# TensorE's experts 1 to 6 as a hardware loop, expert 0's rare tiles moved ahead of it, and the FFN's first block moved into the attention's last wait

## The chip, the core and the metric

The kernel runs on one core of a Trainium2 chip. A core has five engines with instruction streams of their own: TensorE (matmuls, PE in the profile, its weight loads PEld), VectorE (DVE), ScalarE (ACT), GpSimd (POOL) and SyncE (SP, which here only starts DMAs). They meet through semaphores. The metric is the device time of the program in microseconds, from which the median of several executions is taken.

## The reference, cut to what matters

```python
def _attn_ref(r, k, v, w, u):                    # B, H, S, D = 2, 8, 768, 48
    for t in range(S):
        kt, vt, rt = k[:, :, t], v[:, :, t], r[:, :, t]
        cur = einsum('bhd,bhe->bhde', u[None] * kt, vt)
        y[:, :, t] = einsum('bhd,bhde->bhe', rt, state + cur)
        state = w[None, :, :, None] * state + einsum('bhd,bhe->bhde', kt, vt)
...
def _moe_ref(x, w_in, w_out, alpha):             # 1536 tokens, 384 -> 2048 -> 384
    h = x @ w_in
    return (maximum(h, 0.0) + alpha * minimum(h, 0.0)) @ w_out
...
def _moe2_ref(x, w_gate, w1, w2, capacity):      # 8 experts, 384 -> 1024 -> 384
    logits = x @ w_gate; expert_idx = argmax(logits, axis=1)
    # softmax gives the token's gate; the first 384 tokens of each expert are kept
    h = maximum(einsum('ecd,edf->ecf', disp, w1), 0.0)
    y = einsum('ecf,efd->ecd', h, w2)
    # out[i] = gate_w[i] * y[expert_idx[i], pos[i]] for kept tokens, else 0
```

A linear attention with decay, then a dense feed-forward network (FFN, "mlp"), then a mixture of 8 experts ("moe") that takes each token to one expert.

## The kernel before

Every engine's program is written by hand, in one order, with hand-written semaphore waits; nothing schedules it. Three stages follow each other.

**Attention** goes over 12 tiles of 128 tokens (`for t in range(T)` on TensorE). Per tile it turns k (`k_turn`), makes the scores (`scored`), takes the state's part and then the scores' part of the output (`stage2`, lines 1318 and 1326) and updates the state (`update`). The scores' part waits until VectorE has masked the scores (`mask`, line 956), and VectorE until ScalarE has written their diagonals (line 676). The last tile's output is split into a high and a low part by `x_high` and `x_low`.

**FFN.** Every f32 product is made as three fp32r products of high and low parts: high with high, high with low, low with high. Tokens come in 4 groups of 384, the width of 2048 in 16 blocks of 128 (a block is a "chunk" of weights, with 384 columns of w_in and 384 of w_out). `up(g, f)` makes 9 matmuls (line 1359); VectorE makes the leaky relu in two operations (`leaky`, lines 1014 and 1020), ScalarE rounds it to the high part (`g_high`, line 705), GpSimd subtracts (`g_low`, line 551), and `down(g, f)` makes 9 matmuls (line 1374). In group 0 the weights are split too: ScalarE rounds a chunk (`split_high`, line 659), VectorE subtracts its two halves in two operations of `split_low` (line 933). GpSimd has split the first half of chunks 0 to 3 during the attention (EARLY = 4). Groups 1 to 3 are a loop on TensorE (`pe.Fori`), with a body of 316 matmuls.

**Experts.** While the last FFN group ends, 256 early rows of expert 0 go through `early_up` and `early_down`; expert 0 keeps up to 128 more rows. The number of rows of each expert stands in `counts`, and each engine reads it into a register (`rows_of`) and branches on it. An expert has three tiles of 128 rows, and there are three ways through it:

- at most 128 rows: `flip_up` twice (18 matmuls, 512 columns), `flip_turn` (8 transposes), the next expert's rows turned (`turn_xe`, 9 transposes), then `expert_down(e, 0)` with 24 matmuls (line 1593);
- up to 256 rows: `expert_ups` (8 blocks of 9 matmuls, 256 columns, line 1555, with the next expert's 9 transposes between), `expert_down(e, 1)` and `expert_down(e, 0)`;
- more: these and the third tile by `flip_up`, `flip_turn` and `expert_down(e, 2)`.

In this data expert 0 (after its early rows), 5, 6 and 7 go the first way, experts 1, 2 and 3 the second and expert 4 the third. On TensorE the code of all 8 experts is written out one after the other, each with both sides of two branches (If on 128 rows, If on 256 rows), 238 matmuls in an expert. After an expert's tiles, ScalarE scales its outputs by the gate (`y_copy`, line 828) and GpSimd scatters them to `out` with indirect DMAs (`y_scatter`, line 609). GpSimd waits for the scatters of the experts before (`s_out`) and then counts `s_gone` up, which frees `y_out` and `token`. The weights of expert e+2 are loaded and split while e and e+1 run; the first half by ScalarE and GpSimd (lines 798 and 633), the second by ScalarE and VectorE (lines 807 and 1145). The last three chunks of expert 1 (`split_high` and `split_low` of 29 to 31) are split at the end of expert 0's branch.

## Time and profile before

| | us |
|---|---|
| median of 3 runs | 434.99 |
| lowest, highest | 433.43, 435.9 |
| profiled execution, its own time | 433.0 |
| its span, first to last instruction | 431.3 |

The profile is of one execution. In its page, a digit row gives the busy share in 40 slices of the span; groups of instructions have the form "line engine op out<-in xcount | busy, mean of one | idle before, and who ended it".
### The profile page before, as it was taken

How to read it: one execution, taken by the hardware profiler on the slowest of the kernel's cores; microseconds unless marked ns; L12 is line 12 of the kernel's file. 1: busy time of each engine (PE TensorE's matmuls, PEld its weight loads, DVE VectorE, ACT ScalarE, POOL GpSimd, SP SyncE). 2: the span in 40 equal slices, each digit the busy share in tenths (PEclk: the TensorE clock that was granted, in tenths of full speed). 3: DMA queues.
4: the chain of work that ended last, by engine and by line, in shares of the span. 5: the costliest groups of instructions: out<-in, count | busy, mean ns of one | idle time of the engine just before them, and what ended most of it. 6: DMA issues, size and time to landing. Idle time of an engine off the chain costs nothing.

```text
span 431.3 us, 9203 instructions
## 1 busy us (share of the span) xinstructions
PE 407.6 (95%) x3200; PEld 389.3 (90%) x3200; DVE 263.5 (61%) x525; ACT 195.5 (45%) x446; POOL 228.2 (53%) x239
## 2 busy tenths in 40 slices
PE   5799999999999999999999999999699999999892
PEld 5698889999999999999999999987699999998672
DVE  6898867676436334353444796756586695726850
ACT  2889943433311114011142433425668777437840
POOL 3999725554322533126254593142939476437942
PEclk9999999999999999999999999999899999999997
DMA  6996035444990100001000455059575685817400
GB/s 244 403 370 217 3 82 165 131 135 152 362 358 3 53 2 0 0 0 55 0 0 4 129 154 171 18 144 388 176 254 161 234 258 185 277 25 244 140 29 10
DMA packets 34339, 61.89 MB, mean 144 GB/s; under 512 B 4798, under 2 KB 27310, under 8 KB 34288
## 3 DMA queue, kind: packets, MB, share of 16 engines
q1 hardware_dynamic: 31280, 55.92, 39.3%
q0 software_dynamic: 3008, 5.29, 3.6%
q8 instruction: 31, 0.51, 0.5%
q14 instruction: 20, 0.16, 0.1%
HBM read 47.92 MB, written 15.18 MB: 146 GB/s over the span
## 4 chain that ended last, share of the span: by engine, by line
PE 59%; PEld 15%; issue 7%; POOL 5%; DVE 5%; ACT 4%; DMA 2%; PEldq 0%; POOLq 0%; ACTq 0%; DVEq 0%
PE bank L1374 23%; PE bank L1359 23%; PEld bank L1593 7%; PEld bank L1555 6%; ACT scores L676 3%; POOL w_low L633 3%; PE bank L1480 2%; PE bank L1490 2%; DMA out<-y_out,token 2%; PEld bank L1617 1%; PE bank L1326 1%; DVE scores L956 1%; POOL out L609 1%; DVE w_low L1145 1%; PE bank L1617 1%
## 5 line engine op out<-in xcount | busy, mean ns | idle before, releaser
L551 POOL TENSOR_TENSOR g_low<-act_full,g_high 128x384 fp32r<-128x384 f32 x63 | 63.7, 1011 | 113.7 <-ACT g_high L705 113.7
L705 ACT ACTIVATE g_high<-act_full 128x384 fp32r<-128x384 f32 x64 | 33.7, 526 | 148.9 <-DVE act_full L1020 136.3
L1359 PE MATMUL bank<-x_split,w_high 128*128 (+1 forms) x384 | 98.3, 337 | 0.0
L1014 DVE TENSOR_SCALAR neg<-bank,alpha_sb 128x384 f32<-128x384 f32 x64 | 39.3, 614 | 78.0 <-PE bank L1359 78.0
L1359 PEld LDWEIGHTS bank<-x_split,w_high 128*128 128x128 f32 x384 | 69.0, 188 | 0.2 <-issue 0.2
L633 POOL TENSOR_TENSOR w_low<-w_raw,w_high 128x384 fp32r<-128x384 f32 x48 | 50.5, 1086 | 33.5 <-ACT w_high L798 33.5
L1374 PE MATMUL bank<-w_high,g_high 128*128 128x384 f32 x189 | 65.0, 344 | 0.0
L1359 PE MATMUL bank<-x_split,w_low 128*128 (+1 forms) x192 | 64.4, 336 | 0.0
L1374 PE MATMUL bank<-w_high,g_low 128*128 128x384 f32 x189 | 63.8, 338 | 0.0
L1374 PE MATMUL bank<-w_low,g_high 128*128 128x384 f32 x189 | 63.8, 337 | 0.0
L933 DVE TENSOR_TENSOR w_low<-w_raw,w_high 128x384 fp32r<-128x384 f32 x44 | 35.5, 812 | 10.5 <-ACT w_high L659 10.5
L1593 PE MATMUL bank<-w_high,expert_g_high 128*128 128x384 f32 x104 | 35.6, 342 | 2.9 <-DVE expert_g_low L1196 1.8
L1374 PEld LDWEIGHTS bank<-w_high,g_high 128*128 128x128 f32 x189 | 35.4, 187 | 2.1 <-POOL g_low L551 1.0
L1020 DVE SCALAR_TENSOR_TENSOR act_full<-bank,neg 128x384 f32<-128x384 f32 x64 | 35.7, 558 | 2.4
L1359 PEld LDWEIGHTS bank<-x_split,w_low 128*128 128x128 f32 x192 | 36.0, 188 | 0.0
L1374 PEld LDWEIGHTS bank<-w_low,g_high 128*128 128x128 f32 x189 | 35.5, 188 | 0.0
L1374 PEld LDWEIGHTS bank<-w_high,g_low 128*128 128x128 f32 x189 | 35.4, 187 | 0.0
L1593 PE MATMUL bank<-w_high,expert_g_low 128*128 128x384 f32 x104 | 34.8, 335 | 0.0
L1593 PE MATMUL bank<-w_low,expert_g_high 128*128 128x384 f32 x104 | 34.8, 335 | 0.0
L1145 DVE TENSOR_TENSOR w_low<-w_raw,w_high 128x384 fp32r<-128x384 f32 x48 | 33.0, 704 | 0.0
L609 POOL DMA_INDIRECT out<-y_out,token x24 | 26.0, 1082 | 12.5 <-DMA out<-y_out,token 6.7
L1555 PE MATMUL bank<-xe_high,w_high 128*128 128x256 f32 x96 | 28.5, 297 | 2.8 <-issue 2.8
(164 smaller groups left out, 846.3 us busy)
## 6 DMA issues: line engine op xcount, KB each, us to landing
w_raw<-chunks SPq DMA_DIRECT2D x96, 192.0 KB, 4.1
w_raw<-chunks SPq DMA_DIRECT2D x32, 384.0 KB, 3.5
rk_in<-att_rk SPq DMA_DIRECT2D x12, 704.0 KB, 6.4
routed_rows<-fill SPq DMA_DIRECT2D x1, 5211.0 KB, 16.8
xe<-routed_rows SPq DMA_DIRECT2D x7, 579.0 KB, 4.5
v_in<-att_v SPq DMA_DIRECT2D x12, 200.0 KB, 6.1
out<-fill SPq DMA_DIRECT2D x1, 2304.0 KB, 23.4
x_split<-x_split POOLq DMA_DIRECT2D x18, 48.0 KB, 2.5
```

Source lines behind the costliest of these rows:

```text
L551: pool.tensor_tensor(gl[:, f % 4, :], act_full[:, f % 2, :], gh[:, f % 4, :].bitcast(f32), ALU.subtract).then_inc(s_gl, 1)
L609: pool.indirect_dma_start(out=out, out_offset=bass.IndirectOffsetOnAxis(ap=token[:, e % 2, i:i + 1], axis=0), in_=y_out[:, e % 2, i, :], i ...
L633: pool.tensor_tensor(wl[:, slot, 0:W1], raw1[:, f, :], wh[:, slot, 0:W1].bitcast(f32), ALU.subtract).then_inc(s_wl1e, 1)
L705: act.activation(gh[:, f % 4, :], act_full[:, f % 2, :], ACT.Copy).then_inc(s_gh, 1)
L933: dve.tensor_tensor(wl[:, slot, part], raw[:, m, part], wh[:, slot, part].bitcast(f32), ALU.subtract).then_inc(s_wl1 if first else s_wl2, 1)
L1014: dve.tensor_scalar(neg[:, f % 2, :], h, 0.0, alpha_sb[:, f:f + 1], ALU.min, ALU.mult)\
L1020: dve.scalar_tensor_tensor(act_full[:, f % 2, :], h, 0.0, neg[:, f % 2, :], ALU.max, ALU.add)\
L1145: dve.tensor_tensor(wl[:, slot, W1:CW], raw2[:, f, :], wh[:, slot, W1:CW].bitcast(f32), ALU.subtract).then_inc(s_wl2, 1)
L1359: last = mm(bank[f % 4][:, 0:G], a[:, f, w], x[:, kc, bass.ds(g * G, G)], start=kc == 0 and i == 0, stop=kc == KC - 1 and i == 2)
L1374: last = mm(bank[4 + i][:, 0:DM], a[:, f % 4, i * P:(i + 1) * P], w[:, slot, W1:CW], start=f == 0 and m == 0, stop=f == n - 1 and m == 2)
L1555: last = mm(bank[f % 4][:, 0:n], a[:, slot, w], x[:, e % 2, kc, 0:n], start=kc == 0 and i == 0, stop=kc == KC - 1 and i == 2)
L1593: last = mm(bank[4 + i][:, 0:DM], a[:, f, i * P:(i + 1) * P], w[:, s % SLOTS, W1:CW], start=f == 0 and m == 0, stop=f == NFE - 1 and m == 2)
```

## The change

1. **FFN's first block.** On TensorE `up(0, 0)` moves from behind the attention to before `stage2` of its last tile. On VectorE, the first-half split of chunk f+4, done after block f, becomes that of chunk f+3, from block 1 on.
2. **Expert 0.** Its second and third tile, which it has only with more than 128 rows left, get code of their own in front (`flip_up`, `flip_turn` and a new `flip_down` for each), behind one branch that this data skips. Its first tile then stands outside any branch. The rows of tiles 1 and 2 are turned only in the rare branch. The splits of chunks 29 to 31 move ahead of `flip_high` on ScalarE and between the two `flip_relu` on VectorE, and `keep_meta(0)` (the copies of tokens and gates) ahead of the branch.
3. **Loop.** Experts 1 to 6 on TensorE become three turns of a loop over two experts; expert 7 stands behind it. Row numbers are read at the head of each expert (`rows_of`), no longer in `early_down`. Waits now compare with register values.
4. **`flip_down`** takes the place of `expert_down` for a flipped tile and for tile 0 of experts with up to 256 rows: in each half first the 8 products with the high part of g, then the 4 with its low part.
5. **Last scatter.** GpSimd no longer waits for the scatters of experts 0 to 6 before those of expert 7.

```diff
             def load_xe(e):
                 if e >= 2:
-                    sp.wait_ge(s_te, (e - 1) * GT)
+                    sp.wait_ge(s_te, (e - 2) * GT + 1 if e > 2 else 2)
...
-                if e:
+                if 0 < e < E - 1:
                     pool.wait_ge(s_out, e * 16 * GT)
                     pool.sem_inc(s_gone, 1)
...
+            for c in range(2 * NF - 3, 2 * NF):
+                split_high(c)
+            flip_high(0, 0, (0,))
+            xe_high(1, 0, bank[X_BANK[0]])
+            flip_high(0, 0, (1,))
...
-                    if split == "mlp" and f + EARLY < NF:
-                        split_low(f + EARLY, first=True)
+                    if split == "mlp" and EARLY < f + EARLY <= NF:
+                        split_low(f + EARLY - 1, first=True)
...
+                if t == T - 1:
+                    pe.wait_ge(s_par, 32)
+                    pe.wait_ge(s_cast, 1)
+                    pe.wait_ge(s_moved, MOVES)
+                    pe.wait_ge(s_masked, T - 1)
+                    up(0, 0)
                 stage2(t)
...
+            def flip_down_high(e, i, half, b):
+                pe.wait_ge(s_fc[i], 2 * e + half + 1)
+                for f in range(half * HF, (half + 1) * HF):
+                    pe.wait_ge(s_wl2, s + NF + 1)
+                    for w in (wh, wl):
+                        mm(bank[4 + i][:, 0:DM], egh[:, f, i * P:(i + 1) * P], w[:, b * NFE + f, W1:CW],
+                           start=f == 0 and w is wh, stop=False)
...
             early_down(1, 0)
             pe.wait_ge(s_cnti, 2)
-            rows = []
+            rows_0 = rows_of(pe, 0)
             for f in range(1, NFE):
-                rows.append(rows_of(pe, f - 1))
                 early_down(1, f)
-            rows.append(rows_of(pe, E - 1))
...
+            def expert(e, b):
+                rows = rows_of(pe, e)
+                with pe.If(rows < P + 1):
...
+            pe.wait_ge(s_wl1, NF + 2 * NFE)
+            with pe.Fori(1, E - 1, 2) as e:
+                expert(e, 1)
+                expert(e + 1, 0)
+            expert(E - 1, (E - 1) % 2)
```

How instructions stand now. TensorE at the attention's last tile, before: the state's part and the scores' part of tiles 10 and 11, then the FFN's first block.

```order
L1318 MATMUL bank<-r_hat,state 64x128 x8
L1326 MATMUL bank<-scores,v_in 64x128 x8
L1318 MATMUL bank<-r_hat,state 64x128 x8
L1326 MATMUL bank<-scores,v_in 64x128 x8
L1359 MATMUL bank<-x_split,w_high 128x384 x2
```

And now, at the same place:

```order
L1354 MATMUL bank<-r_hat,state 64x128 x8
L1362 MATMUL bank<-scores,v_in 64x128 x8
L1378 MATMUL bank<-x_split,w_high 128x384 x2
L1378 MATMUL bank<-x_split,w_low 128x384
...
L1354 MATMUL bank<-r_hat,state 64x128 x8
L1362 MATMUL bank<-scores,v_in 64x128 x8
```

The nine matmuls of `up(0, 0)` now stand between tile 10's output and both parts of tile 11's.

VectorE in expert 0, the branch that this data takes, before (L933 is `split_low` of chunks 29 to 31):

```order
L1190 TENSOR_SCALAR expert_g_by_token<-bank 128x512
L1151 TENSOR_TENSOR xe_low<-bank,xe_high 128x3x128
L1159 CAST token<-xe 128x3
L1160 COPY gate<-xe 128x3
L1190 TENSOR_SCALAR expert_g_by_token<-bank 128x512
L1196 TENSOR_TENSOR expert_g_low<-bank,expert_g_high 128x4x128
L1151 TENSOR_TENSOR xe_low<-bank,xe_high 128x3x128
L1196 TENSOR_TENSOR expert_g_low<-bank,expert_g_high 128x4x128
L1151 TENSOR_TENSOR xe_low<-bank,xe_high 128x3x128 x2
L933 TENSOR_TENSOR w_low<-w_raw,w_high 128x384 x3
```

And now (L953 is `split_low`):

```order
L1214 TENSOR_SCALAR expert_g_by_token<-bank 128x512
L953 TENSOR_TENSOR w_low<-w_raw,w_high 128x384 x3
L1214 TENSOR_SCALAR expert_g_by_token<-bank 128x512
L1220 TENSOR_TENSOR expert_g_low<-bank,expert_g_high 128x4x128
L1174 TENSOR_TENSOR xe_low<-bank,xe_high 128x3x128
L1220 TENSOR_TENSOR expert_g_low<-bank,expert_g_high 128x4x128
L1174 TENSOR_TENSOR xe_low<-bank,xe_high 128x3x128 x2
L1182 CAST token<-xe 128x3
```

The three splits went from behind both halves of g into the middle between them, and the copies of expert 0's tokens out of this stretch.

TensorE at the loop's end and the start of expert 7 behind it:

```order
L1792 UNCONDITIONAL_BRANCH
L1802 REGISTER_ALU
L1802 COMPARE_AND_BRANCH
L321 TENSOR_LOAD counts
L321 ISA x2
L1768 COMPARE_AND_BRANCH
L1701 MATMUL bank<-w_high,xe_high 128x512
```

The load of a row number now stands right in front of the branch that uses it, at the head of each expert; TensorE's program has four such loads, where before it had eight in `early_down`.

## Rows read from the trace of the kernel before

**Rows 1.** The page, section 1: busy us, share of the span, instructions

```profile
PE 407.6 (95%) x3200; PEld 389.3 (90%) x3200; DVE 263.5 (61%) x525; ACT 195.5 (45%) x446; POOL 228.2 (53%) x239
```

**Rows 2.** Windows from:to, us; busy PE, PEld, DVE, ACT, POOL; PEclk; DMA; GB/s

```profile
306.90:310.70 3.80, 3.76 (x19) 3.79 (x20) 1.34 (x2) 0.80 (x2) 3.80 (x5) 0.57 0.66 196
...
326.30:344.10 17.80, 17.80 (x130) 17.80 (x129) 13.40 (x25) 13.33 (x33) 11.44 (x12) 1.00 0.70 221
```

**Rows 3.** Timeline of PE at the attention's end: start, us, line, operation, idle before

```profile
55.92 1.09 PE L1318 MATMUL bank<-r_hat,state 64*64 64x128 f32 x16
58.07 1.09 PE L1326 MATMUL bank<-scores,v_in 128*64 128x128 f32 x16 [1.05 <-DVE scores L956]
59.09 0.62 PE L1359 MATMUL bank<-x_split,w_high 128*128 128x384 f32 x2
```

**Rows 4.** The chain that ended last, in FFN group 0: start, us, what

```profile
59.16 8.01 PE bank L1359 x45
67.17 5.02 PE bank L1374 x27
...
73.75 1.62 PE bank L1374 x9
...
105.63 1.59 PE bank L1374 x9
```

**Rows 5.** Timeline of DVE, then of ACT, in FFN blocks 0 and 1

```profile
61.03 0.62 DVE L1014 TENSOR_SCALAR neg<-bank,alpha_sb 128x384 f32<-128x384 f32 x1 [0.51 <-PE bank L1359]
...
63.69 0.62 DVE L933 TENSOR_TENSOR w_low<-w_raw,w_high 128x384 fp32r<-128x384 f32 x1 [0.98 <-ACT w_high L659]
...
62.81 0.85 ACT L659 ACTIVATE w_high<-w_raw 128x768 fp32r<-128x768 f32 x1
```

**Rows 6.** Timeline of PE in `early_down`, around two reads of row numbers

```profile
284.25 0.33 PE L1490 MATMUL bank<-w_high,expert_g_low 128*128 128x384 f32 x1
284.58 0.41 PE L1490 MATMUL bank<-w_high,expert_g_high 128*128 128x384 f32 x1
```

**Rows 7.** Timeline of PE at the start of expert 0

```profile
289.37 0.82 PE L1522 MATMUL bank<-ident,xe 128*128 128x128 f32 x6
...
291.59 0.47 PE L1617 MATMUL bank<-w_high,xe_high 128*128 128x512 f32 x1 [0.35 <-DVE xe_low L1151]
```

**Rows 8.** Timeline of PEld from expert 0's down products to expert 1

```profile
298.32 0.19 PEld L1593 LDWEIGHTS bank<-w_high,expert_g_high 128*128 128x128 f32 x1 [0.40 <-issue]
...
302.82 0.19 PEld L1593 LDWEIGHTS bank<-w_high,expert_g_high 128*128 128x128 f32 x1 [1.40 <-issue]
...
306.91 0.19 PEld L1555 LDWEIGHTS bank<-xe_high,w_high 128*128 128x128 f32 x1 [3.10 <-issue]
```

**Rows 9.** DMA queues, window 160 to 266 us (all three), then 300 to 303 us

```profile
q1 hardware_dynamic: 1598, 4.03, 13.5%
q0 software_dynamic: 384, 1.19, 2.9%
q14 instruction: 1, 0.01, 0.0%
...
q8 instruction: 1, 0.02, 2.2%
```

**Rows 10.** Timeline of PE, first matmul of expert 6

```profile
401.50 0.47 PE L1617 MATMUL bank<-w_high,xe_high 128*128 128x512 f32 x1 [1.25 <-issue]
```

**Rows 11.** Timeline of PE, first down products of experts 6 and 7

```profile
408.56 0.41 PE L1593 MATMUL bank<-w_high,expert_g_high 128*128 128x384 f32 x1 [0.68 <-DVE expert_g_low L1196]
...
419.18 0.41 PE L1593 MATMUL bank<-w_high,expert_g_high 128*128 128x384 f32 x1 [0.66 <-DVE expert_g_low L1196]
```

**Rows 12.** Timeline of ACT and of POOL at the end

```profile
423.72 0.58 ACT L828 ACTIVATE y_out<-bank,gate 128x384 f32<-128x384 f32 x1 [3.54 <-PE bank L1593]
...
425.43 0.97 POOL L609 DMA_INDIRECT out<-y_out,token  x1 [0.31 <-issue]
```

**Rows 13.** Timeline of DVE, the splits of chunks 29 to 31

```profile
300.51 3.93 DVE L933 TENSOR_TENSOR w_low<-w_raw,w_high 128x384 fp32r<-128x384 f32 x3
```

361 lines of the change are left out of this document (219 added, 142 removed).

## The prediction

> **What bounds the kernel now.** I read the shares of the engines first, then windows over the stages, the chain that ended last, and the timelines at each place that the diff touches. TensorE is busy 95% of the span, the next engine 61% [rows 1]. In a stage without gaps it is busy all the time: expert 2 keeps it for 17.80 of 17.80 us, with VectorE at 13.40, ScalarE at 13.33, GpSimd at 11.44 [rows 2]. So the time is TensorE's work plus TensorE's gaps, and behind it the last scatter. The change removes hardly any matmul; what it can win is the gaps. The gaps of about half a microsecond or more on the path are: the wait for the last mask [rows 3], two reads and a handover around expert 0 [rows 6, 7], three gaps with no releaser but "issue" [rows 8, 10], and waits of the flipped experts for the low part [rows 11]. Each other engine has slack, so a shift of TensorE's work carries on to the end unless one of the rivals below holds it.
>
> **The FFN's first block.** TensorE ends the state's part of tile 11 at 57.0 and waits until 58.07 for the mask [rows 3]. `up(0, 0)` costs 45 matmuls / 8.01 us, so 1.6 us for 9 [rows 4]. Put in front at 55.9, it ends at 57.5, the state's part (1.0) at 58.5: the scores' part starts 0.4 later than the 58.07 of before. One block of 1.6 less, 0.4 later: 1.2 won by there, if the block's inputs are in; its weights and its tokens have been ready for microseconds. Then VectorE: `leaky(0)` stood at 61.03, behind the split of the last tile's output, and can't be much earlier. Block 4's first-half split ended at 64.3 (63.69 + 0.62) [rows 5]; now it stands behind `leaky(1)` and another split, at about 65.0, and `up(4)`, ready to start at 64.3, waits for it. It starts 0.6 earlier than before (65.0 against 67.17 - 1.56). So 0.6 by block 4. After that the cycle of before goes: VectorE waited 0.98 for ScalarE's rounding of the same chunk [rows 5] in every block, and TensorE's down products came at 1.62 us per 9 there against 1.59 at the group's end [rows 4]. 10 blocks at 0.03, and the 27 products of 5.02 that need only 27 x 0.177 = 4.8: 0.5 more. **1.2 us** in all (1.1 to 1.3 by either way of counting; 0 if the wait that takes the place of the old one is as long as the block).
>
> **Reads of row numbers.** TensorE's matmuls of 384 columns follow at 0.17 us, but 284.25 to 284.58, across a read, is 0.33 [rows 6]. The first reads hide behind queued work, the last four show 0.16 to 0.2 each, and one at the end 0.3: **0.8 us** gone. They come back at the head of six loop experts and of expert 7. One read and its branch against a queue of work that, by the way the first four hide, is about a microsecond deep: I take 0.1 each, **0.5 us** in all; the ends are 0 and 0.6 each (0.77 us per block with a read, less 6 instructions that take a part of it), 4.2 in all. The Trainium skill ("Runtime: NRT & Kernel Launch", section "Instruction fetch mechanics") puts a register load at some 200 ns; by that figure, as an estimate, seven unhidden reads would be 1.4 us. The sum stays with the rows.
>
> **Expert 0's start.** Six transposes stood before the last six early products, 0.82 us [rows 7]; three stay: 0.3. Expert 0 began at 291.59, 0.5 after the last product, because it waited for both tiles' low parts [rows 7]; for one tile the wait is about 0.2: 0.3. Three more transposes go in its middle (0.4). Against that, VectorE makes the three splits between the halves of g. They took 3.93 us for three beside GpSimd [rows 13], 0.55 each alone. The second half's relu then comes 0.6 to 2 us after TensorE has run out of transposes. I take 0.6, net of the 0.4: 0.2 lost. Together **0.4 us** won; at the long splits 1 lost.
>
> **Code gaps.** PEld stood still 1.40 us in the middle of expert 0's down products and 3.10 before expert 1 [rows 8]. The last split that expert 1 could wait for ended at 304.4 [rows 13], and the gap at 301.4 to 302.8 had no input outstanding. In the first a packet of the instruction queue q8 lies just before the restart [rows 9]. I read these as blocks of code that had not come. After them the granted clock was 0.57 for 3.80 us [rows 2], a loss of 0.43 x 3.8 = 1.6. The same kind of gap, 1.25, stands before expert 6 [rows 10]. What tells whether the change removes them: a block is 16 KB; a matmul is two instructions [rows 1], and expert 0 jumped over 105 matmuls into a block, ran through its rest in 2 to 4 us while the weights of expert 2 were loading, and jumped on. By my count of the code the next block was asked for only at the first jump. In the changed kernel the jump comes 8 us earlier, before expert 0's tile, so the next block has 10 us to come; then each block of the loop is in use for 5 us or longer in the first turn. And in turns two and three nothing need be fetched: FFN groups 2 and 3 run from 160 to 266 us and q8 moves nothing at all in them, only a single packet of q14 [rows 9], though their body has 316 matmuls. The expert body has 476, half as much again. Gone: 1.1 + 2.9 + 1.6 = 5.6 and 1.25 before expert 6: **6.9 us**.
>
> The skill's same section says the opposite of what this change banks on: that instruction memory is a short sequential buffer with no benefit from locality, and that a taken branch out of its window stalls. The trace does not agree with it for 316 matmuls [rows 9]; for 476 no row here tells, and the rule is the rival for slower below. The same section gives TensorE's memory as 128 KiB, eight such blocks, which would hold the body.
>
> **High products first.** Before, the flipped experts' down products waited for VectorE's low part: 0.68 and 0.66 us [rows 11], and 0.27 in expert 5. Now eight products of high parts (1.4 us) come first, and ScalarE's part is ready 0.7 earlier. **1.6 us.** Nothing is late in its place: the low part is there 0.7 into the 1.4.
>
> **The end.** The last y tile is copied at 423.72 to 424.30, the last scatter begins 1.1 later [rows 12], since GpSimd was held by the wait for expert 6's scatters. Without that the scatter needs about 0.8 from the copy to its start: **0.3 us.** GpSimd's own row of scatters (1.28 each) could bind when TensorE ends some 3 us earlier relative to it; by my count it is 0 to 0.5 us from doing so.
>
> **Sum**, against the profiled execution's 433.0 us (span 431.3, 1.7 around it): -1.2 - 0.8 + 0.5 - 0.4 - 6.9 - 1.6 - 0.3 = -10.7, so 422.3. That execution lay 2 us under the median of the runs shown, 434.99; a gain of 2.5% puts the median at **424.2 us**.
>
> **Rivals.**
>
> *The code gaps stay, at other places.* Two jumps in a row are still there, with weights loading, at the entry of the loop and at the exit to expert 7. For it: before, three of the eleven such places stalled, all with weights loading. Against it: the count of code above. If the 6.9 stay whole: 424.2 + 6.9 = 431.1. If one gap of 2.9 stays with its clock loss: 428.7.
>
> *The loop's bookkeeping shows.* Seven reads at 0.6 and a register operation for each wait: 424.2 + 3.7 = 427.9. For it: every wait in the body now has such an instruction, often one for two matmuls. Against it: FFN groups 1 to 3 use such waits with no gap, if fewer of them.
>
> *The other engines don't follow.* VectorE's splits beside GpSimd at 1.3 us each cost expert 0 another 1.4 [rows 13] and the front block wins nothing (1.2): 424.2 + 2.6 = 426.8.
>
> *Slower: the body doesn't stay in instruction memory.* It is half as long again as the one that does. Then each return to the top is a jump to a block that isn't there, and the next jump, over the short branch, to another. From [rows 8], a landing costs 3.10; two are 6.2, and 1.6 for the clock: 7.8 per return, 15.6 for two, against 6.9 banked, and the forward jumps of later turns stall as well where they now don't. 424.2 + 15.6 = 439.8. It decides as soon as the engine keeps fewer than the five or six blocks of this body; four are shown. This is the mechanism that ends above the time of before.
>
> **How the numbers follow.** Forecast 0.58; gaps at other places 0.13; bookkeeping 0.11; others don't follow 0.08; slower 0.10. A measurement of this kernel tells about 0.5% (2.2 us) from no change. The forecast's own range, from the bounds of the reads, the splits and the block, is 421.5 to 427; the rivals short of the slower one reach 431.1. Leaving out the slower one and the full stay of the gaps gives 421.2 to 430.5. Faster by over 0.5%: the first four cases less a little for two of them meeting, 0.87; same 0.04; slower 0.09.
>
> **What would show it.** In the changed profile: the FFN's chain begins with 36 matmuls of the up line behind the last scores' part, and its down groups read 1.59 early on; the products of `early_down` follow at 0.17 without gaps but one; no "issue" gap over 0.5 us on PEld between expert 0 and expert 1 and no window there below clock 1.00; no packet of q8 between the loop's second turn and its end; the first product of flipped experts' downs waits under 0.2 us; the last scatter begins under 0.9 us after the last copy. The prediction is wrong if q8 is busy in turns two and three, or if "issue" gaps stand at each expert's head, or if a DVE line ends TensorE's waits in expert 0 for over a microsecond.

## The result, and the profile after

| | before | after |
|---|---|---|
| median of 14 runs, us | 435.14 (433.43 to 435.9) | 431.12 (429.56 to 433.11) |
| profiled execution, us | 433.0, span 431.3 | 429.56, span 427.9 |
| granted clock, mean | 0.991 | 0.996 |

The ratio is 0.9925, with a 95% interval of 0.9911 to 0.994. The change is 0.75% faster; 2.5% were forecast. The direction was right, the size was not: 431.12 lies outside the range of 421.2 to 430.5.

The page's first section after, as [rows 1] of before, and the row of instruction packets from the page's third (queue, kind: packets, MB, share):

```profile
PE 406.9 (95%) x3194; PEld 388.8 (91%) x3195; DVE 258.3 (60%) x523; ACT 192.6 (45%) x442; POOL 229.8 (54%) x239
...
q8 instruction: 22, 0.36, 0.3%
```

TensorE has six transposes fewer. Its busy time falls by 0.7 us and its idle time by 2.7 (431.3 - 407.6 = 23.7 us before, 427.9 - 406.9 = 21.0 after). Where the 3.4 us went is read from the first product of each expert in TensorE's timelines:

| first product of | before | after | ahead of before |
|---|---|---|---|
| expert 0 | 291.59 | 289.65 | 1.94 |
| expert 1 (two tiles) | 306.94 | 300.91 | 6.03 |
| expert 2 (two tiles) | 326.45 | 318.85 | 7.60 |
| expert 3 (two tiles) | 344.36 | 338.33 | 6.03 |
| expert 4 (three tiles) | 362.31 | 357.82 | 4.49 |
| expert 5 (one tile) | 389.43 | 386.51 | 2.92 |
| expert 6 (one tile) | 401.50 | 397.13 | 4.37 |
| expert 7 (one tile) | 412.79 | 409.85 | 2.94 |
| span's end | 431.3 | 427.9 | 3.4 |

Up to expert 2 the forecast is nearly kept: 7.6 us won. Then each of experts 2, 3 and 4 gives back some 1.55 us, and in expert 6 another 1.43 of the 1.45 that its start had won goes. The first product of experts 1 and 3, and of the down in expert 2 (TensorE's timeline: start, duration, line, operation, idle before):

```profile
300.91 0.28 PE L1600 MATMUL bank<-xe_high,w_high 128*128 128x256 f32 x1
...
329.88 0.44 PE L1631 MATMUL bank<-w_high,expert_g_high 128*128 128x384 f32 x1 [0.55 <-DVE xe_low L1174]
...
338.33 0.28 PE L1600 MATMUL bank<-xe_high,w_high 128*128 128x256 f32 x1
```

Ahead of expert 1 there is no gap any more, where before there were 3.10 [rows 8]. But from expert 1 to 2 are 17.94 us, from 2 to 3 19.48 and from 3 to 4 19.49, where before the last two were 17.91 and 17.95 (the first was 19.51, with the lower clock of [rows 2] in it). What stands before expert 2's relus is seen on ScalarE. First before, in the same place one expert later, then after (ScalarE's timeline; the first row of each is `flip_high` of the expert that ends, the last the first relu of the next):

```profile
339.87 1.09 ACT L843 ACTIVATE expert_g_high<-bank 128x512 fp32r<-128x512 f32 x2 [2.73 <-PEq L1681]
340.84 1.77 ACT L798 ACTIVATE w_high<-w_raw 128x384 fp32r<-128x384 f32 x4
...
345.63 0.38 ACT L790 ACTIVATE expert_g_high<-bank 128x256 fp32r<-128x256 f32 x1
```

```profile
315.91 1.09 ACT L848 ACTIVATE expert_g_high<-bank 128x512 fp32r<-128x512 f32 x2 [4.31 <-PEq L1791]
316.88 1.77 ACT L801 ACTIVATE w_high<-w_raw 128x384 fp32r<-128x384 f32 x4
...
321.58 0.40 ACT L793 ACTIVATE expert_g_high<-bank 128x256 fp32r<-128x256 f32 x1
```

Before, the relu starts 1.27 us behind the next expert's first product (345.63 - 344.36), which is about when its block is made. After, it starts 2.73 us behind it (321.58 - 318.85). What released `flip_high` is line 1791, `pe.sem_inc(s_ft[2], 2)`: a count which says that the third tile's halves are turned, raised without work where there is no third tile (line 1681 before, where the same count was `s_ft[1]`). Before, TensorE raised it after 15 of the 24 products of the first tile's down. The change rewrote the down as `flip_down` and put the count behind all 24:

```diff
-                    expert_down(e, 0, range(HF + 1))
-                    pe.wait_ge(s_mgl, e * NFE + NFE + C_MGL)
-                    pe.sem_inc(s_ft[1], 2)
-                    expert_down(e, 0, range(HF + 1, NFE))
+                    flip_down(e, 0, b)
+                    pe.sem_inc(s_ft[2], 2)
```

Nine products of 0.173 us are 1.56 us. In a two-tile expert ScalarE runs `flip_high(e, 2)` all the same, on data nobody uses, and behind it stand its splits of the next W1 and its copies of y: 5.67 us (315.91 to 321.58) from there to the next relu. The late count of one two-tile expert so delays the relus of the expert behind it: those of experts 1, 2 and 3 lengthen experts 2, 3 and 4.

### The profile page after: what moved, and what is told of

The parts are those of the page before. It is cut to its first block, busy times and chain, and to the rows that moved or that the text cites. A ratio compares the mean times of both kernels' runs of the same rounds, so it can differ in the third digit from the quotient of the medians.

```text
span 427.9 us, 9352 instructions
## 1 busy us (share of the span) xinstructions
PE 406.9 (95%) x3194; PEld 388.8 (91%) x3195; DVE 258.3 (60%) x523; ACT 192.6 (45%) x442; POOL 229.8 (54%) x239
## 4 chain that ended last, share of the span: by engine, by line
PE 69%; DVE 9%; issue 5%; PEld 5%; POOL 4%; DMA 3%; ACT 2%; SPq 0%; PEldq 0%; POOLq 0%; ACTq 0%; DVEq 0%
PE bank L1417 24%; PE bank L1378 23%; POOL w_low L636 4%; PE bank L1362 3%; PE bank L1701 3%; DVE w_low L1165 3%; PE bank L1326 3%; PE bank L1354 2%; PE bank L1651 2%; PE bank L1631 2%; PEld bank L1600 2%; PEld bank L1631 2%; DMA w_raw<-chunks 2%; PE bank L1312 1%; DVE expert_g_low L1158 1%
## 5 line engine op out<-in xcount | busy, mean ns | idle before, releaser
L554 POOL TENSOR_TENSOR g_low<-act_full,g_high 128x384 fp32r<-128x384 f32 x63 | 65.2, 1035 | 111.2 <-ACT g_high L708 111.2
L1165 DVE TENSOR_TENSOR w_low<-w_raw,w_high 128x384 fp32r<-128x384 f32 x48 | 33.5, 714 | 0.0
L953 DVE TENSOR_TENSOR w_low<-w_raw,w_high 128x384 fp32r<-128x384 f32 x44 | 31.2, 736 | 0.2 <-ACT w_high L662 0.2
L679 ACT ACTIVATE scores<-ident,diag 128x128 f32<-128x128 f32 x96 | 29.4, 398 | 2.4 <-DVE diag L968 2.4
L662 ACT ACTIVATE w_high<-w_raw 128x768 fp32r<-128x768 f32 x32 | 26.8, 838 | 2.6 <-DMA w_raw<-chunks 2.6
L1600 PE MATMUL bank<-xe_high,w_low 128*128 128x256 f32 x96 | 27.1, 282 | 0.0
```

Source lines behind the costliest of these rows:

```text
L554: pool.tensor_tensor(gl[:, f % 4, :], act_full[:, f % 2, :], gh[:, f % 4, :].bitcast(f32), ALU.subtract).then_inc(s_gl, 1)
L662: act.activation(wh[:, slot, :], raw[:, m, :], ACT.Copy).then_inc(s_wh, 1)
L679: last = act.activation(scores[:, t % 2, h % 2, h // 2, :], ident[:, :], ACT.Copy, scale=diag[:, t % 2, h:h + 1])
L953: dve.tensor_tensor(wl[:, slot, part], raw[:, m, part], wh[:, slot, part].bitcast(f32), ALU.subtract).then_inc(s_wl1 if first else s_wl2, 1)
L1165: dve.tensor_tensor(wl[:, slot, W1:CW], raw2[:, f, :], wh[:, slot, W1:CW].bitcast(f32), ALU.subtract).then_inc(s_wl2, 1)
L1600: last = mm(bank[f % 4][:, 0:n], a[:, slot, w], x[:, b, kc, 0:n], start=kc == 0 and i == 0, stop=kc == KC - 1 and i == 2)
```

## The experiments

Ratios are to the kernel before, run beside each group on the same chip. Spans and starts are of each kernel's profiled execution.

**x1: the count first.**

```diff
-                    no_tile(2)
-                    flip_down(e, 0, b)
-                    pe.sem_inc(s_ft[2], 2)
+                    pe.sem_inc(s_ft[2], 2)
+                    no_tile(2)
+                    flip_down(e, 0, b)
```

> Theory A (a count that comes too late): in the changed kernel TensorE raises the count for the third tile's halves (s_ft[2]) of a two-tile expert after all 24 products of the first tile's down, nine products of 0.17 us later than the kernel before did; ScalarE's copies, its split of the next W1, GpSimd's half of that split, VectorE's keep_meta and so the next expert's first relu stand behind it. Here the count is raised ahead of those 24 products. By A the distance between the starts of two-tile experts falls from 19.5 to about 17.9 us for experts 2, 3 and 4, and the whole run is 3 x 1.6 = 4.7 us shorter than the change: 426.4 us, range 424 to 428, a ratio of 0.980 to the kernel before. Rival B (the loop's registers: TensorE computes its waits from registers in every turn, and that costs the 1.6 us per expert): nothing moves, 431 us, and the starts stay 19.5 us apart. Rival C (the two-tile experts wait for the weights' load or split, not for this count): 431 us too, with the wait of VectorE's keep_meta gone but one of a weight's in its place.

Measured 427.06 us, ratio 0.9805 (0.9776 to 0.9833), span 424.4. The distances are 17.94, 17.91 and 17.95. By the two ratios the one line moved gives 1.2% of the time; by that of x5 below, which executes the same instructions and came to 0.9848, it gives 0.8%. Either is as much as the whole change had. ScalarE at the end of expert 2:

```profile
330.02 1.09 ACT L848 ACTIVATE expert_g_high<-bank 128x512 fp32r<-128x512 f32 x2 [0.57 <-PEq L1789]
```

It starts 6.66 us ahead of expert 3's first product (336.68), where after it started 2.94 ahead of expert 2's. Expert 3's first relu then starts 1.27 us behind the first product, as in the kernel before, and now ScalarE waits 0.40 for TensorE there: 1.27 is the earliest that it can be. Rivals B and C fall. Not all of the gain lasts: x1 is 4.76 us ahead of the changed kernel at expert 5 (381.75 against 386.51) and 3.5 at the span's end, because expert 6 takes 13.61 us in x1 and 12.72 in the changed kernel. x6 below says why.

**x2: the kernel before with the count last.**

```diff
-                    expert_down(e, 0, range(HF + 1))
-                    pe.wait_ge(s_mgl, e * NFE + NFE + C_MGL)
-                    pe.sem_inc(s_ft[1], 2)
-                    expert_down(e, 0, range(HF + 1, NFE))
+                    expert_down(e, 0)
+                    pe.sem_inc(s_ft[1], 2)
```

> The kernel before with nothing changed but the place of the same count: after all 24 products of the first tile's down instead of after 15. Theory A: experts 2, 3 and 4 take 1.6 us more each, so 435.1 + 4.7 = 439.8 us (438 to 441), ratio 1.011, with the starts of the two-tile experts about 19.4 us apart instead of 17.9. Rival B (the loop's registers) and rival C (weights): no change, 435.1 us.

Measured 439.56 us, ratio 1.0078 (1.0058 to 1.0098). The distances from 2 to 3 and 3 to 4 are 19.42 each. So the late count costs the old kernel as well, with no loop in it. The three experts take 1.51, 1.47 and 1.53 us more, 4.5 together; the medians differ by only 3.1. The kernel before was at 436.45 in this group of runs and at 434.4 to 435.3 in the others, so what the medians say is itself known to a microsecond or so only; no run says more of the rest.

**x3 and x4: no loop**, with the count last and first.

```diff
-            with pe.Fori(1, E - 1, 2) as e:
-                expert(e, 1)
-                expert(e + 1, 0)
-            expert(E - 1, (E - 1) % 2)
+            for e in range(1, E):
+                expert(e, e % 2)
```

> The change with its loop written out (each expert's code stands once, with constants in its waits), all else kept, the late count too. Theory A: the two-tile experts' starts stay 19.5 us apart, and the three stops for code and the clock drop come back: +6.9 us less what the waits behind the late count take of them (up to 3 us), so 435 to 438 us, ratio 1.000 to 1.007. Rival B: the registers' cost goes with the loop, the two-tile experts take 17.9 us again and the code gaps come back: 431.1 - 4.7 + 6.9 = 433.3 us.

> The loop written out and the count raised ahead of the 24 products. Theory A: against the first run of this set (426.4) only the code stops come back, +6.9 us: 433.3 us (431.5 to 434.5), ratio 0.996; the difference of this run and the first is the value of the loop by itself. If the loop's worth is less than forecast (the stops for code were in part cover for other waits), this one comes out at 430 or lower. Rival B: the same 433.3, but then the first run stays at 431, so that the loop is worth only 2 us.

Measured 432.4 us, ratio 0.9923 (0.9896 to 0.9949), and 426.9 us, ratio 0.9793 (0.9771 to 0.9816). Forecast were 435 to 438 us and 433.3. Both are as fast as their partners with the loop (0.9925 and 0.9805). This is the surprise of the study: the forecast's largest term was put down to the loop, and the loop is not needed for most of it. The trace of x4 has no stop before expert 1, whose first product is at 301.66, right behind expert 0's last, and the clock stays at 1.00. Of the three stops of before only the one ahead of expert 6 is there:

```profile
395.23 0.47 PE L1701 MATMUL bank<-w_high,xe_high 128*128 128x512 f32 x1 [1.77 <-POOL w_low L636]
```

This row names GpSimd's split, but x1's expert 6, with the same splits, starts without a wait; two instruction packets of x4 lie in these microseconds, none of x1. Nor was the split late. The eight splits of expert 6's first half end with this row of GpSimd's timeline in x4, at 386.03, 7 us before the stop begins (393.46):

```profile
384.01 2.02 POOL L636 TENSOR_TENSOR w_low<-w_raw,w_high 128x384 fp32r<-128x384 f32 x2 [0.34 <-ACT w_high L801]
```

I read it as a stop for code under a wrong name. The loop's own worth is 0.7 us of span (425.1 against 424.4), and nothing that the timing can tell. Its registers cost nothing: expert 1 takes 17.94 with them, 17.93 without. The reads at the experts' heads cost nothing either: experts 2 and 3 take 17.91 and 17.95 in x1, with a read in front of each, as in the kernel before, which has none there. A window from 340 to 410 us of the changed kernel holds these DMA queues and no q8, whereas x4's same window holds eight packets of it (and five of q14):

```profile
q1 hardware_dynamic: 7967, 11.02, 51.4%
q0 software_dynamic: 704, 1.05, 4.0%
q14 instruction: 4, 0.03, 0.2%
```

```profile
q8 instruction: 8, 0.13, 0.8%
```

So the loop's body is not fetched again. Only, the fetches had been nearly free.

**x5 and x9: code that is never run, laid into expert 0** of x1's kernel. x5 had the condition `rows_0 < 0`, which was decided when the program was built, so its blocks were left out: 427.31 us, ratio 0.9848 (0.9822 to 0.9874), and nothing learned of code. But it shows what one program does in two executions, since x5 and x1 run the same 9352 instructions: ratios of 0.9848 and 0.9805, spans of 425.4 and 424.4, a wait in expert 0 of 1.46 us and of 0.59, and 18.17 us from expert 2 to 3 and 17.91. A difference of a microsecond between two spans is therefore no finding here. x9:

```diff
             flip_turn(0, 0, (1,))
+            with pe.If(rows_0 < P + 1):
+                pe.wait_ge(s_tel, 1)
+            with pe.Else():
+                keep_warm(105)
             flip_down(0, 0)
+            with pe.If(rows_0 < P + 1):
+                pe.wait_ge(s_tel, 1)
+            with pe.Else():
+                keep_warm(74)
```

> The first run of the study (loop kept, count raised first) with two stretches of code that is never run laid into expert 0: 105 transposes between its second turn and its down, 74 transposes between its down and expert 1. The kernel before jumps over as much code at these two places. Theory D (where expert 0's rare code stands, not the loop, took the two stops and the clock's drop away, as the run without the loop suggests: it has no stop there): both stops come back, about 1.1 us before expert 0's down and 2.9 us before expert 1, and expert 1 runs 1.6 us longer at the lower clock, +5.6 us on 427.1: 432.7 us (430.5 to 433.5), ratio 0.993. Rival E (it is the loop that took them away, by the code that it brings in or keeps): no change, 427.1 us, ratio 0.981.

> The fifth run again, with a condition that is only known when the program runs (the fifth one's could be decided when it was built, so its two blocks were left out of the program): in expert 0 of the first run's kernel TensorE now jumps over 105 transposes ahead of its down and over 74 behind it. Theory D (the place of the code in front of these two points made the two stops of the kernel before): 1.1 us before the down and 2.9 us before expert 1 come back, with the clock's drop behind them 5.6 us: 432.7 us, ratio 0.993. Rival E (what made them was something else of expert 0's old form, or the loop took them away): 427 to 427.5 us, ratio 0.982.

x9 took 440.12 us, ratio 1.0117 (1.0077 to 1.0157): 13 us more than x1, where 5.6 were forecast, though all that it executes besides is two tests and two waits that hold at once. The first product of expert 1 and the first of expert 7's down, and the clock behind the first stop and at the second (windows; busy PE, PEld, DVE, ACT, POOL; PEclk, DMA, GB/s):

```profile
306.35 0.38 PE L1600 MATMUL bank<-xe_high,w_high 128*128 128x256 f32 x1 [3.30 <-POOL w_low L636]
...
423.89 0.66 PE L1651 MATMUL bank<-w_high,expert_g_high 128*128 128x384 f32 x1 [4.02 <-issue]
```

```profile
306.90:310.30 3.40, 3.40 (x18) 3.40 (x17) 0.97 (x2) 0.92 (x3) 2.95 (x4) 0.50 0.77 219
...
422.90:429.70 6.80, 5.81 (x18) 5.84 (x19) 0.00 (x0) 0.58 (x1) 1.12 (x2) 0.50 0.02 3
```

The stop before expert 1 and the half clock behind it are back (the one before expert 0's down is not). A stop of 1.31 has come before expert 2, and one of 4.02 in expert 7, whose code nobody touched but which now lies elsewhere, with 6.8 us at half clock from within it. Against x1, expert 0 takes 4.9 us more, expert 1 3.1 and expert 7 6.0. The loop is in both kernels, so it is not what decides; that it is the place of code and not the two tests themselves, the next pair shows.

**x13 and x14: the kernel before, with never-run code some 20 us ahead of expert 0.**

```diff
                 early_down(1, f)
+                if f == 2:
+                    with pe.If(rows[0] < P + 1):
+                        pe.wait_ge(s_cnti, 2)
+                    with pe.Else():
+                        keep_warm(102)
```

> The kernel before with nothing changed but never-run code (102 transposes and the branch around them, 208 instructions) laid between two of its early downs, some 20 us ahead of expert 0, so that all code behind it lies 208 instructions further on. Theory D2 (the stops depend on where the jumps fall among the packets of instructions, about 256 instructions each by the profile's count of packets and MB, not on the loop or the order): by the distances, expert 0's second jump then no longer leaves the packet it starts in, so the stop before expert 1 (2.81 us) and the clock's drop behind it (1.6 us) go: 435 - 4.4 = 430.5 us (429 to 432), ratio 0.990. Rival E2 (the old form of expert 0 makes the stops wherever it lies): both stops stay, 435 us, ratio 1.000.

> The same with 51 transposes (106 instructions). By theory D2 both jumps of expert 0 still leave the packet that they start in, as in the kernel before, so the stops stay: 435 us, ratio 0.997 to 1.004; stops of other experts may shift. If the stop goes here as well, the distance of the packets isn't what decides, and some other property of the shift is. Rival E2: 435 us.

With 102 transposes: 433.41 us, ratio 0.9953 (0.9934 to 0.9972). With 51: 441.07 us, ratio 1.012 (1.0101 to 1.014). In the first, forecast at 430.5, the 2.81 before expert 1 are 0.71 and the clock doesn't drop, as expected; the 1.11 in expert 0's down are gone too, which was not; but new stops stand before a down of expert 1 (0.88), in expert 2 (0.89) and before expert 3 (0.59), so only a part is won. In the second I expected no change and was wrong: stops of 2 us and more at four places, of which one, expert 0's down, had 1.11 before and the others (in experts 5, 6 and 7) had none for code. Three of the four:

```profile
301.81 0.41 PE L1593 MATMUL bank<-w_high,expert_g_high 128*128 128x384 f32 x1 [3.23 <-issue]
...
400.50 0.33 PE L1593 MATMUL bank<-w_high,expert_g_high 128*128 128x384 f32 x1 [2.91 <-issue]
412.13 0.41 PE L1593 MATMUL bank<-w_high,expert_g_high 128*128 128x384 f32 x1 [3.40 <-DVE w_low L1145]
```

Both execute the same, a branch and a wait more than the kernel before, and differ only in how many never-run transposes lie there: 433.4 against 441.1 us. That the place of code decides is shown. The rule by which I placed it (a stop where a jump leaves its packet soon after the last one did) got one of the two right, and that one in part, and stays a guess.

**x6, x7 and x8: VectorE's order.** `keep_meta(e)` stood at the end of expert e-1 and waits there for GpSimd's scatters. x6 (count first) and x7 (count last) move it into expert e; x8 is x6 with the splits between two relus put behind both.

```diff
                         for i in range(1, GT):
                             xe_low(e + 1, i, bank[X_BANK[i]])
+                    if e > 1:
+                        keep_meta(e)
...
-                if e < E - 1:
-                    keep_meta(e + 1)
```

x8 has besides:

```diff
                     flip_relu(e, 0, 0)
-                    low2(0, 1)
                     flip_relu(e, 0, 1)
-                    low2(2)
+                    low2(0, 1, 2)
```

> Count raised first, and VectorE's keep_meta(e) moved from the end of expert e-1 into expert e (behind its halves' low parts in a one-tile expert, behind the eight relus in a two-tile one), from expert 2 on. In the trace of the first run VectorE stands 1.09 us before keep_meta ahead of expert 6 and takes 0.81 and 1.06 us for it, and TensorE's wait for its relu (1.21 us) follows. Theory A extended (keep_meta is the gate by which the scatter holds the relus): 1.2 us of TensorE's wait in expert 6 go and some of the 0.85 us: 425.6 us (424.5 to 426.5), ratio 0.977. Rival F (VectorE's weight splits, not keep_meta, bound experts 5 to 7): no change, 427 us.

> The change as it was measured, the count raised after the 24 products as there, with keep_meta(e) moved into expert e. Theory A says that the late count costs time only by way of keep_meta: VectorE's next relu stood behind it. So with the count late and keep_meta out of the way the starts of the two-tile experts should come back from 19.5 to about 17.9 us, and the time to that of the run before this one, within 0.5 us: 425.6 to 426.5 us, ratio 0.978. Rival G (the late count holds something else also, ScalarE's copy or GpSimd's split of the weights, which TensorE needs itself): 428 to 431 us, with starts 18.5 to 19.5 us apart.

> As the sixth run (count first, keep_meta later), and in one-tile experts, expert 0 among them, VectorE's weight splits that stood between its two relus (three in expert 0, two in the others) follow both relus. TensorE waited for the second relu 0.59 us in expert 0 and 0.85 us in expert 6 in the first run's trace, where these splits took 2.12 us. If VectorE's order bounds these experts, 1 to 1.5 us more go: 424.4 us (423.5 to 425.5), ratio 0.974. If the splits are then late for the next product that reads them, the same as the sixth run.

x6: 426.93 us, ratio 0.9834 (0.9803 to 0.9866), span 423.5 against x1's 424.4. Expert 6 takes 12.02 us instead of 13.61, so the wait was real, but the timing can't tell the 0.9 us (425.6 us were forecast). x8: 425.47 us, ratio 0.9788 (0.9771 to 0.9805), span 423.2, where 424.4 us were forecast. x7 corrects my theory: 429.62 us, ratio 0.9894 (0.9864 to 0.9924), distances of 19.02 and 19.04. With the count last and `keep_meta` out of the way only 0.45 of the 1.55 us per expert come back. So ScalarE's own queue is the main way in which the late count acts: in x7's expert 2 VectorE's first `relu_low` (which makes the low part of g) waits 4.19 us for ScalarE's relu.

```profile
324.35 0.42 DVE L1158 SCALAR_TENSOR_TENSOR expert_g_low<-bank,expert_g_high 128x256 fp32r<-128x256 f32 x1 [4.19 <-ACT expert_g_high L793]
```

**x17 and x18: how much of the delay counts.** x17 is the change with the count after 20 of the 24 products (between `flip_down_high(e, 0, 1, b)` and `flip_down_low(e, 0, 1, b)`); x18 is the kernel before with it ahead of all 24.

> The change with the count raised after 20 of the 24 products (the last four, the second half's low parts, follow it) instead of after 24. If ScalarE's queue sets the distance product by product, each of the starts of experts 3, 4 and 5 comes 4 x 0.173 = 0.69 us sooner after the one before (18.8 us instead of 19.5), 2.1 us in all: 431.1 - 2.1 = 429.0 us, ratio 0.9876 (0.985 to 0.990). If a threshold decides (a DMA caught or missed), the distance is either 17.9 or 19.5 us.

> The kernel before with the count raised ahead of the 24 products instead of after 15 of them. In its trace ScalarE's first relu of expert 3 starts 1.27 us after the expert's first product, which is 0.2 us later than in the first run's kernel, and TensorE does not wait: the count came just in time. So nothing is gained: 435.3 us, ratio 0.997 to 1.003, starts 17.9 us apart as before. If it gains over 1 us, the count was holding the kernel before too.

x17: 430.0 us, ratio 0.9888 (0.9865 to 0.9911), distances 18.80 and 18.83: 0.68 us less for four products of 0.173. x18: 435.29 us, ratio 1.001 (0.9992 to 1.0028), distances 17.92 and 17.95: nothing. Both as expected. (The expectation calls the relu 0.2 us later than in x1; x1 has the same 1.27.) The cost over 17.91 us is 1.57 behind 24 products, 0.89 behind 20 and nothing behind 15 or ahead of all. At 0.173 each that puts the last place that costs nothing, by estimate, at the 15th, and from there on each product is paid in full, once per expert.

**x10, x11 and x15: a one-tile expert's down inside the branch of its turns.** In x10 the product rows follow the turns without a second test of the row count. A two-tile expert's first tile takes `expert_down` again in all three. x11 adds x8's moves; x15 is x11 with 70 never-run transposes as in x13.

```diff
                     flip_turn(e, 0, (1,))
+                    pe.sem_inc(s_w1free, 1)
+                    pe.sem_inc(s_fh[2], 2)
+                    pe.sem_inc(s_ft[2], 2)
                     no_tile(1)
+                    no_tile(2)
+                    flip_down(e, 0, b)
                 with pe.Else():
...
-                with pe.If(rows < 2 * P + 1):
+                    with pe.If(rows < 2 * P + 1):
```

> The first run's kernel with a one-tile expert's down written inside the same branch as its turns, instead of behind a second test of the row count (the two-tile and the three-tile ways stand in the other branch). In the first run's trace TensorE idles 0.71 to 0.74 us between the last turn and the first product of the down in experts 6 and 7, and 0.38 us in expert 5, though the halves' high parts are there; in expert 0, whose down follows without a branch, no such gap shows. Theory H (the gap is the branch and the register waits behind it): 0.38 + 0.74 + 0.71 = 1.8 us less, of which the low parts of the halves may take back up to 0.8: 425.6 us (425 to 426.5), ratio 0.977. Rival I (the gap is ScalarE's copy of the first half): 427 us.

> The tenth run's kernel with the eighth's two moves on VectorE as well (keep_meta in the expert itself, the splits behind both relus). If the waits that each takes away are separate ones, their gains add up: 427.1 - 1.8 - 2 = 423.3 us, ratio 0.970 (422.5 to 424.5). If experts 5 to 7 are bound by the same chain in both, 424.5 to 425.5 us as the eighth.

> The eleventh run's kernel with 70 never-run transposes at the same place, so that the jumps of experts 1 and 2 leave a packet once instead of twice. Theory D2: the stop of 1.27 us before expert 2 goes and nothing else changes: 426.55 - 1.3 = 425.2 us, and its span 422.9 instead of 424.2. If another stop appears, the same or more.

x10: 427.06 us, ratio 0.9828 (0.9796 to 0.986), where 425.6 were forecast. The gap before the down, 0.53 in expert 7 of the changed kernel and 0.71 in x1, is 0.20 now (0.39 in expert 6); but the new code has a stop of 2.32 before expert 2, in the loop's first turn only. The first product of expert 7's down in the changed kernel and in x10, and x10's expert 2:

```profile
416.10 0.41 PE L1651 MATMUL bank<-w_high,expert_g_high 128*128 128x384 f32 x1 [0.53 <-issue]
```

```profile
323.29 0.38 PE L1600 MATMUL bank<-xe_high,w_high 128*128 128x256 f32 x1 [2.32 <-POOL w_low L636]
...
415.41 0.41 PE L1651 MATMUL bank<-w_high,expert_g_high 128*128 128x384 f32 x1 [0.20 <-issue]
```

x11: 426.55 us, ratio 0.9819 (0.9784 to 0.9854), stop of 1.27 at the same place, span 424.2; the two forecasts, 423.3 and 424.5 to 425.5, both fail. x15: 425.08 us, ratio 0.9771 (0.9752 to 0.9791), span 422.9: the stop is gone, and the 1.3 us of span are what was expected, if hardly more than the 1.0 between x1 and x5. It is the fastest of the study, 2.3% under the kernel before and, by the ratios, 1.5% under the change. x8, without any of this, is within its interval.

**x12: x1 without the FFN's part.** The first up block stands behind the attention again and VectorE's splits a block earlier, as before.

> The first run's kernel without the FFN's part of the change (the first up block stands behind the attention again, and VectorE splits W1 a block earlier). In the trace after the change the FFN's second group starts 0.84 us earlier than before. If that lasts to the end, this one takes 0.8 us more than the first run: 427.9 us, ratio 0.9825 (0.980 to 0.985), with group 1's first product at 107.2 instead of 106.4. Rival: the FFN's downs wait for something else, and nothing is lost, 427.1 us.

Measured 426.95 us, ratio 0.9823 (0.9784 to 0.9861): with such an interval the timing says nothing of 0.8 us, nor does the span, 425.0 against 424.4. In the traces the FFN's group 1 starts at 107.62 against 106.55 (106.86 in x5) and expert 0 at 290.87 against 289.81 (290.13), so there the block's gain is seen.

**x16: x1 with the plain order of products** in the loop and expert 7 (`expert_down(e, 0, b)` for `flip_down(e, 0, b)`).

> The first run's kernel with the plain order of products (high, low, low in turn) in experts 5 to 7; expert 0 keeps the new order. The forecast gave the new order 1.6 us in all, of 0.66 to 0.68 us waits before a down and one at expert 0. The trace after the change shows 0.4 to 0.7 us before the same downs still. If the order is worth its forecast, this one takes 0.27 + 0.68 + 0.66 = 1.6 us more, 428.7 us; if the gap is the branch and not the data (theory H), nothing changes: 427.1 us, ratio 0.9805.

Measured 428.41 us, ratio 0.9853 (0.9825 to 0.9882), span 425.7 against 424.4. The number is near the 428.7 that a full worth of the order gives, but the trace doesn't bear that out. The gap at expert 6's down is what it was with the new order:

```profile
403.27 0.44 PE L1631 MATMUL bank<-w_high,expert_g_high 128*128 128x384 f32 x1 [0.74 <-DVE expert_g_low L1220]
```

Of the 1.3 us 0.76 arise in expert 0, whose code is the same in both kernels, and the rest in experts 2 to 4, not at the places where I had put it. x5, with the new order, has just these longer times in experts 0 and 2 to 4, and its span is only 0.3 us under x16's. So the order is worth 0.5 us at most, and perhaps nothing.

## Why the prediction missed

The sum again, term by term, with what the traces show (us, minus is a gain).

| term | forecast | measured | |
|---|---|---|---|
| FFN's first block | -1.2 | -0.8 | group 1 starts at 106.38, not 107.22 |
| reads, and expert 0's start | -0.8, part of -0.4 | -1.1 | 1.94 at expert 0's start less the 0.8 |
| reads at the experts' heads | +0.5 | 0 | 17.91 and 17.95 in x1 as before |
| stops at expert 0 and the clock | -5.6 | -5.7 | 4.09 in expert 0, 1.57 in expert 1 |
| stop before expert 6 | -1.25 | -1.45, then +1.43 | VectorE's waits take its place |
| high products first | -1.6 | 0 to -0.5 | |
| the end | -0.3 | -0.3 to -0.5 | 1.38 from last copy to last scatter, not 1.71 |
| the count raised later | no term | +4.7 | 1.57, 1.54 and 1.57 in experts 2, 3 and 4 |

**The step that failed is one that is missing.** The list of edits called the new down an order of products. The same lines also moved a count from behind 15 products to behind 24, and neither the description nor the prediction has it. "Nothing is late in its place" was said of the low part, on TensorE alone. Who waits for TensorE was not asked. The trace of before had what was needed: ScalarE's `flip_high` released by that line after 2.73 us, 5.76 us from there to its next relu with no idle time between, and that relu 1.27 us after the expert's first product. There was no room. "Each other engine has slack" was read from ScalarE's share, 13.33 of 17.80 us [rows 2], and not at this place. With the term in it the sum is -6.0 instead of -10.7, and 424.2 + 4.7 = 428.9. Of the 2.2 us that are still missing, expert 6 has 1.2, the order of products 1.1 or more and the FFN's block 0.4, less the 0.5 for reads that cost nothing. One of the rivals, that the gaps for code stay at other places in full, gives 431.1 us, which is what was measured. That is chance: in this kernel those gaps are gone, and the count took their gain.

**High products first** was mis-sized. The 0.68 and 0.66 of [rows 11] name VectorE's low part, and I took the name for the cause. In x16 and x1 the gap at expert 6 is 0.74 with either order; in x10, where the second test of the row count no longer lies in it, it is 0.20 at expert 7 and 0.39 at expert 6. I read it so that the low part arrived while the branch was still being worked off: two things ended there at nearly the same time, and the row names one.

**The stop before expert 6** went as forecast, and nothing came of it. VectorE had been just behind: `keep_meta(6)`, held by the scatters, then the relu, then two splits between the relus. After, TensorE waits for the relus of expert 6:

```profile
401.88 0.63 PE L1722 MATMUL bank<-ident,expert_g_by_token 128*128 128x128 f32 x4 [0.46 <-DVE expert_g_by_token L1214]
...
404.28 0.66 PE L1722 MATMUL bank<-ident,expert_g_by_token 128*128 128x128 f32 x4 [0.79 <-DVE expert_g_by_token L1214]
...
405.56 0.44 PE L1651 MATMUL bank<-w_high,expert_g_high 128*128 128x384 f32 x1 [0.62 <-DVE w_low L1165]
```

x6 and x8 take that chain away, and expert 6 takes 12.02 and 12.06 us in them, not the 13.61 of x1. x4 shows it the other way round: with the 1.77 stop back ahead of expert 6, experts 5 and 6 together take 24.34 us, and 24.43 in x1 without it. The prediction asked what is late next for the products, not for this stop.

**The FFN's block** won 0.84 of 1.2. `up(4)` waits for VectorE as said and starts at 65.07, 0.54 earlier than before; 0.6 was forecast. Behind it 0.30 came of 0.5. The rows are of the chain that ended last, as [rows 4]:

```profile
56.19 1.77 PE bank L1378 x9
...
65.07 1.86 PE bank L1378 x9
66.93 4.77 PE bank L1417 x27
...
73.26 1.59 PE bank L1417 x9
```

The 27 products take the 4.77 that were worked out (5.02 before), and the blocks' downs 1.59 each (1.62 before). What the sum forgot is that `up(4)`, having to wait, takes 1.86 us for the 1.56 of its neighbours.

**What held.** The three stops were read as code that had not come; x9, which brings the one before expert 1 back by code that is never run, bears that out. The 5.6 us around expert 0 came to 5.7. The reason given for the two at expert 0 (the jump comes 8 us earlier, so that the next block has time) did not need the loop, and x3 and x4 agree with it; but x13 and x14 say that it is one lucky place among others. The rival that the code gaps go to other places, given 0.13, is no rival of this kernel but the general case: x9, x10, x11 and x14 each met it. The loop's bookkeeping cost nothing. The slower rival fell: 476 matmuls of loop body are fetched once and then kept, no packet of q8 from the second turn on. The rule of the Trainium skill ("Runtime: NRT & Kernel Launch", section "Instruction fetch mechanics"), that the memory is a short sequential buffer with nothing to gain from locality, doesn't hold for this loop on TensorE; the 128 KiB that the same section gives for TensorE's memory leave room for the body, and the trace agrees. Its warning that a taken branch out of the window stalls the engine fits the stops of x9 and x14, 1.3 to 4.0 us each; but x4 jumps over the unused branches of every expert and stops once.

**Expert 0's splits.** The wait for the second relu was put at 0.6. It is 0.83 in the changed kernel and between 0.59 and 1.73 in kernels with the same code there (x1, x4, x9, x10, x16); x1 and x5, the same instructions twice, have 0.59 and 1.46. x8, which has the splits behind both relus, has 0.33 before the first product of the down and no wait between the halves. Such a spread is itself larger than several terms of the sum, and no run says where it comes from.

## What to carry to other kernels

When an edit rewrites a stretch of an engine's program, list every semaphore that the stretch raises and the product after which it did so before and does now; then read from the other engine's timeline how much work it has between that count and the next thing the first engine needs. A wait that is removed pays only if the engine which would be late next has slack at that very place. A gain or a loss of one or two per cent from an edit that also moves code should be checked against the same kernel with never-run code laid ahead, before it is put down to the edit.

## What the runs showed of the hardware

- Code that is never run, by its amount, changed the time of one kernel from 435.3 to 433.4 or 441.1 us (x13, x14). Single stops where TensorE jumps cost 0.6 to 4.0 us. Which ones stop and which don't, I could not derive from the distances.
- A loop body of 476 matmuls (some 950 instructions by two each) runs its later turns without a packet of q8, while the same experts written out (x4) fetch eight in the same 70 us, mostly without a stop.
- The granted clock fell to its lower level, 0.50 (1.2 of 2.4 GHz), for 3.4 us after the stop of 3.30 us in x9, and to 0.53 over 3.5 us after the one of 3.40 in x14. It fell again within the stop of 4.02 in x9 (0.50 from 422.9 to 429.7) and within the one of 2.02 in x14 (0.50 from 426.6 to 429.9). After the 2.32 of x10 and the 3.23 of x14 at expert 0's down it stayed at 1.00, and so it did behind the 1.70 before expert 1 in x14, 6 us after the 3.23. In x9 a wait of 1.73 had come 8 us ahead of the first drop's stop, in x14 one of 2.91 12 us ahead; but ahead of the 4.02 TensorE was busy for 8.87 of 9.00 us (410 to 419). What decides isn't shown.
- What I read as a stop for code can carry the name of a split: in x4 and x10 the splits that the product needs had ended 7 and 11 us before the stop began (386.03 for 393.46, 309.69 for 320.97), and in x9 the line named before expert 1 splits expert 2's weights. The end of the right split, the packets of q8 beside the stop, and a run with the same code at another place, tell.
